# Attention and two mixing blocks in one launch: ScalarE makes both bias tables, TensorE gets idle products, one load goes to ScalarE's queue

## The reference

```python
scores = scale * q @ k.T                       # scale = 1/8
keep   = is_global | is_local                  # key < 8, or 0 <= rel < 96
dist   = where(is_global & ~is_local, n_local, abs(rel))
bias   = -slopes[h] * dist                     # slopes[h] = 2 ** -(h + 1) for 8 heads
a      = softmax(where(keep, scores + bias, -1e9))
x      = a @ v                                 # (2, 768, 512) over all heads
u  = x + (V.T @ (U.T @ x))                     # mixing along the sequence, rank 32
x  = u + relu(u @ w_ch1) @ w_ch2               # 512 -> 2048 -> 512
h  = relu(x @ w_in); gate, vv = halves(h)      # 512 -> 1024
out = (gate * (w_spatial @ norm(vv) + b)) @ w_out
```

## Time and profile before

| | us |
|---|---|
| Median of three runs | 530.94 |
| Lowest and highest | 528.90 and 530.97 |
| The profiled execution | 530.2 |
| Its span | 528.4 |
| PE busy | 515.6 |
| DVE busy | 191.3 |
| ACT busy | 181.7 |
| POOL busy | 125.4 |

### The profile page before, as it was taken

One profiled execution on the slowest core, in us unless ns is written; L12 is line 12 of the kernel. 1 busy time (PEld: TensorE's weight loads), 2 busy tenths in 40 slices (PEclk: granted clock), 3 DMA queues, 4 the chain that ended last, 5 costly groups with the idle time before them and its releaser, 6 DMA issues.

```text
span 528.4 us, 7432 instructions
## 1 busy us (share of the span) xinstructions
PE 515.6 (98%) x2808; PEld 440.7 (83%) x2808; DVE 191.3 (36%) x538; ACT 181.7 (34%) x446; POOL 125.4 (24%) x120
## 2 busy tenths in 40 slices
PE   4999999999999999999999999999999999999997
PEld 4799979888788888888888888888888998888996
DVE  6566667722123423121111312112375355440440
ACT  4677788742323321021101233222443212332121
POOL 6477678334333500000000043323000000000000
PEclk8599999999999999999999999999999999999999
DMA  8540641003223210000000022230000000110002
GB/s 241 179 137 2 198 163 42 2 5 117 81 87 111 81 40 1 0 1 1 1 0 1 0 81 89 60 120 19 1 1 2 0 1 0 61 40 21 1 20 99
DMA packets 12245, 27.85 MB, mean 53 GB/s; under 512 B 2225, under 2 KB 2225, under 8 KB 12209
## 3 DMA queue, kind: packets, MB, share of 16 engines
q1 hardware_dynamic: 10480, 24.22, 14.2%
q10 hardware_dynamic: 1728, 3.15, 1.6%
HBM read 24.22 MB, written 3.15 MB: 52 GB/s over the span
## 4 chain that ended last, share of the span: by engine, by line
PE 94%; POOL 2%; DVE 1%; issue 1%; DMA 1%; ACT 0%; DVEq 0%; POOLq 0%; ACTq 0%
PE bank L988 28%; PE bank L1175 25%; PE bank L1163 25%; PE bank L1038 7%; PE bank L1008 4%; PE bank L1021 3%; PE bank L1045 1%; POOL w_slot L421 1%; DVE bias L495 1%; PE bank L1070 1%; PE bank L1059 1%; DMA cfg_i<-in_cfg 1%; POOL qk_split L382 0%; ACT prob L787 0%; DVE qk_split L492 0%
## 5 line engine op out<-in xcount | busy, mean ns | idle before, releaser
L1175 PE MATMUL bank<-hid,w_slot 128*128 128x512 f32 x576 | 139.2, 390 | 0.0
L1163 PE MATMUL bank<-u_split,w_slot 128*128 128x512 f32 x576 | 138.4, 389 | 0.0
L1175 PEld LDWEIGHTS bank<-hid,w_slot 128*128 128x128 f32 x576 | 107.7, 188 | 23.2 <-issue 0.9
L1163 PEld LDWEIGHTS bank<-u_split,w_slot 128*128 128x128 f32 x576 | 107.7, 188 | 22.4
L659 DVE SCALAR_TENSOR_TENSOR hid<-bank,hid 128x512 fp32r<-128x512 f32 x48 | 33.2, 691 | 192.3 <-ACT hid L885 192.3
L885 ACT ACTIVATE hid<-bank 128x512 fp32r<-128x512 f32 x48 | 28.7, 598 | 203.4 <-PE bank L1163 203.4
L787 ACT ACTIVATE prob<-prob,row_min 128x256 f32<-128x256 f32 (+1 forms) x96 | 45.8, 479 | 18.4 <-DVE row_min L510 18.4
L421 POOL TENSOR_TENSOR w_slot<-stage,w_slot 128x1024 fp32r<-128x1024 f32 x16 | 38.2, 2388 | 52.3 <-ACT w_slot L841 52.3
L988 PE MATMUL bank<-sp_slot,vn 128*128 128x384 f32 x288 | 50.3, 334 | 0.0
L988 PEld LDWEIGHTS bank<-sp_slot,vn 128*128 128x128 f32 x288 | 50.0, 188 | 0.2
L1038 PEld LDWEIGHTS bank<-v_all,probT 128*128 128x128 f32 x352 | 43.2, 198 | 2.6 <-issue 1.8
(11 more groups left out here) (89 smaller groups left out, 455.7 us busy)
## 6 DMA issues: line engine op xcount, KB each, us to landing
stage<-in_w_ch SPq DMA_DIRECT2D x16, 512.0 KB, 3.3
qk_raw<-in_qk SPq DMA_DIRECT2D x24, 256.0 KB, 4.5
v_all<-in_v SPq DMA_DIRECT2D x12, 256.0 KB, 5.1
out_dram<-o_stage ACTq DMA_DIRECT2D x12, 256.0 KB, 2.0
stage<-in_w_spT SPq DMA_DIRECT2D x6, 384.0 KB, 3.0
stage<-in_w_in SPq DMA_DIRECT2D x4, 512.0 KB, 3.3
stage<-in_w_out SPq DMA_DIRECT2D x2, 512.0 KB, 3.5
V_raw<-in_V SPq DMA_DIRECT2D x4, 96.0 KB, 4.1
```

The lines of the kernel that those rows point to most:

```text
L1163: last = mm(h_bank[g % 2][:], w_slot[f][:, a, k * P:(k + 1) * P], u_split[c][:, m, k, :], start=(k == 0 and p == 0), stop=(k == KD - 1 and ...
L1175: last = mm(c_ring[(KD * c + k) % 6][:], w_slot[f][:, a, 512 + k * P:512 + (k + 1) * P], hid[g % 2][:, m, :], start=(f == 0 and a == HI an ...
```

## The change

1. ACT makes `bias0` too (eight activations with `dist0` as input), each with its own signal `bias0_set`. DVE does only the two splits. 2. ACT makes the wide `bias` tables two at a time inside its loop: heads 0 and 1 ahead of `exps(0)`, 2 and 3 behind `exps(1)`, 4 and 5 ahead of `exps(2)`, 6 and 7 ahead of `exps(3)`. `score_bias` waits for the tables that it reads. 3. PE does five idle products ahead of `turn(0)` and two more between its pairs. 4. The first half of q and k of block 0 is loaded from ACT's queue as ACT's first instruction, ahead of the table load, and no longer from SP's.

```diff
@@ sync
-                for hq in range(2):
+                for hq in range(1 if t == 0 else 0, 2):
                     c = slice(2 * hq, 2 * hq + 2)
                     sp.dma_start(qk_raw[r][:, c, :, :], qk[t, :, c, :, :]).then_inc(qk_in[r][hq], 16)
@@ vector
-            vec.tensor_scalar(dist[:, 0:GLOB], far[:, 0:GLOB], n_local, None, ALU.add).then_inc(dist_set, 1)
+            vec.tensor_scalar(dist[:, 0:GLOB], far[:, 0:GLOB], n_local, None, ALU.add)
             dve.drain()
             vec.tensor_copy(dist0[:, GLOB:], dist[:, P + GLOB:])
-            vec.tensor_tensor(dist0[:, 0:GLOB], dist[:, P:P + GLOB], dist[:, 0:GLOB], ALU.min)
-            dve.drain()
+            vec.tensor_tensor(dist0[:, 0:GLOB], dist[:, P:P + GLOB], dist[:, 0:GLOB], ALU.min).then_inc(dist0_set, 1)
             for hq in range(2):
                 c = slice(2 * hq, 2 * hq + 2)
                 dve.wait_ge(qk0_hi, hq + 1)
                 vec.tensor_tensor(qk_split[:, LO, c, :, 0:P], qk_raw[0][:, c, :, :],
                                   qk_split[:, HI, c, :, 0:P].bitcast(F32), ALU.subtract).then_inc(qk0_lo, 1)
-                for h in range(4 * hq, 4 * hq + 4):
-                    vec.tensor_scalar(bias0[:, h, :], dist0[:], -(2.0 ** -(h + 1)) / SCALE, None, ALU.mult)
-            dve.drain()
             def score_bias(g):
-                if g == 2:
-                    dve.wait_ge(bias_set, 1)
                 dve.wait_ge(scored, g + 1)
                 for m in range(2):
+                    if g < 2:
+                        dve.wait_ge(bias0_set, heads(g, m)[1][1] + 1)
+                    elif g < 4:
+                        dve.wait_ge(bias_set, heads(g, m)[1][1] + 1)
@@ scalar
+            act.dma_start(qk_raw[0][:, 0:2, :, :], qk[0, :, 0:2, :, :]).then_inc(qk_in[0][0], 16)
             act.wait_ge(ident_set, 2)
             sc.activation(tiny[:, 0:1], ident[:, 0:1], ACT.Exp)
...
-            act.wait_ge(dist_set, 1)
+            act.wait_ge(dist0_set, 1)
             for h in range(H):
-                last = sc.activation(bias[:, h, :], dist[:], ACT.Copy, scale=-(2.0 ** -(h + 1)) / SCALE)
-            last.then_inc(bias_set, 1)
+                sc.activation(bias0[:, h, :], dist0[:], ACT.Copy, scale=-(2.0 ** -(h + 1)) / SCALE
+                              ).then_inc(bias0_set, 1)
+
+            def set_bias(first):
+                for h in range(first, first + 2):
+                    sc.activation(bias[:, h, :], dist[:], ACT.Copy, scale=-(2.0 ** -(h + 1)) / SCALE
+                                  ).then_inc(bias_set, 1)
...
+                    if s in (-2, 0, 1):
+                        set_bias((0, None, 4, 6)[s + 2])
                     if 0 <= s + 2 < QUADS:
                         exps(s + 2)
+                    if s == -1:
+                        set_bias(2)
@@ tensor
-            for _ in range(WARM):
-                mm(aux[:, 0:P], ident[:], ident[:], start=True, stop=True)
+            def fill(count):
+                for _ in range(count):
+                    mm(aux[:, 0:P], ident[:], ident[:], start=True, stop=True)
+            fill(WARM)
...
             def turn(g):
                 for m in range(2):
+                    if g == 0 and m == 1:
+                        fill(2)
                     pe.wait_ge(expd, 2 * g + m + 1)
...
                 for s in range(-2, QUADS):
+                    if s == 0:
+                        fill(5)
```

More of the change, by code:

```diff
@@ L155, in build @@
         cfg_in, b_in, U_in, V_in = [sem(n) for n in ("cfg_in", "b_in", "U_in", "V_in")]
-        counted, V_round, fold_set, dist_set = sem("counted"), sem("V_round"), sem("fold_set"), sem("dist_set")
+        counted, V_round, fold_set = sem("counted"), sem("V_round"), sem("fold_set")
         z_some, z_copy = sem("z_some"), sem("z_copy")
+        dist0_set, bias0_set = sem("dist0_set"), sem("bias0_set")
         bias_set, iotas, ident_set, V_split = sem("bias_set"), sem("iotas"), sem("ident_set"), sem("V_split")
```

## The result

The changed kernel takes 522.28 us (four runs, 522.26 to 522.32) against 530.96 for the kernel before (528.90 to 530.99): 8.7 us less, a ratio of 0.984 with a 95% interval of 0.982 to 0.986. I had forecast 524.9 and a range of 523.4 to 529.0.

The account below looks back on a forecast made before the run. PE was taken to bound the kernel, leaving its start and clock to gain: 3.5 us from the start plus 3.0 from the clock, less 0.3 for `cfg`, is 6.2; 524.7 on the runs' scale, taken as 524.9, range 523.4 to 529.0.

Parts of the forecast that it names:

- The first exponential: Start of ACT's exponentials: moves from 12.88 to 9.4 us, a gain of 3.5 us (bounds 2.4 to 4.3).
- the branch on ACT is hidden in the trace of before; DVE's 1.59 is the nearest row: Reading two numbers and branching ahead of the wide tables: priced at 1.59 us, bounds 1.0 and 2.0.
- The start of ACT's tables: ACT's narrow tables start at 5.4 us, when `dist0` is ready, and end at 7.1 after 1.7 us.
- The second split behind POOL: In rival "The start gains little" (chance 0.18): DVE's second split waits for POOL's subtraction, first exponential gains 2.3, 529.0 us.
- The first load: Block 0's load on ACT's queue: issues 0.43 us earlier, gains nothing; delays `cfg` by 0.3 us (0 to 0.8).
- The stages 0 to 2: With a high clock ACT bounds them; `turn(3)` starts at 21.8 instead of 28.32 us, a gain of 6.5.
- The 0.45 for the two products at the low clock: Idle products between `turn(0)`'s pairs: at the low clock they take 0.78 us and lose 0.45.
- The clock: PE's clock stays high for most of stages 0 to 2, 3.0 us of the gain; forecast case, chance 0.43.
- short stretch at the low level: A short low-clock stretch is likely somewhere, so 524.9 us was taken instead of 524.7.
- The clock falls again: Rival, chance 0.33: low clock in the first stages as before, gain 3.05 to 5, about 526.8 us.
- the two reasons given for a high clock: Ahead of `turn(0)`: 1.1 to 1.9 us of dense idle products; PE's pause shrinks from 5.14 to under 1.5 us.
- The slower case: Rival, chance 0.06: ACT's added work leaves PE gaps in stages 0 to 3, clock rises late; 533.6 us.

Follow-up runs that it names:

- The two drain experiments: Changed kernel with drains of VectorE and ScalarE ahead of the branch: 523.65 us; kernel before without VectorE's drain, a signal per narrow table instead: 529.11 us.
- the runs of 532.5 and 524.5 us at a high clock: Kernel before plus seven idle products, one run of ten: 532.5 us; changed kernel with all wide tables ahead of the first exponential, one of four: 524.48 us.

## Why the prediction was wrong in size

*The first exponential: mis-sized by the branch.* The step that failed is "the branch on ACT is hidden in the trace of before; DVE's 1.59 is the nearest row". DVE's row was measured behind a drain; both new queues have none, and the sequencer does the reading and branching beside the running instructions, so the term is nothing. Both bounds that I kept, 1.0 and 2.0, left zero out. The two drain experiments show it from both sides: with drains the first exponential comes 1.5 us later and the time grows by 1.4, and in the kernel before it comes 1.2 us earlier without one, with 1.6 us less between the last table and the scored heads.

*The start of ACT's tables: wrong the other way.* The first exponential came at 8.26 us instead of 9.4, 1.15 us and not 1.6 sooner, because a second error hid a part of the first. I let the tables start at 5.4, when `dist0` is ready, and wrote that `dist0` comes behind both casts of ACT. It comes behind their starts only: the second cast began at 5.32 us and the wide tables at 5.85. In the changed kernel the tables go on from the second cast at about 6.0, so this term was 0.6 us too small. The rest of that sum held: a narrow table on ACT takes 1.69 / 8 = 0.21 us, two wide ones 0.61. The gain of 4.6 us lies above my bounds for it, 2.4 to 4.3.

*The second split behind POOL: did not happen, but it can.* In the changed kernel the two splits took 1.36 us side by side, with no table between, and POOL's copy beside the second took 1.08 us instead of 0.6. In the kernel before with seven products the second split began after POOL's subtraction and was held up as that rival said:

```profile
7.00 1.76 DVE L492 TENSOR_TENSOR qk_split<-qk_raw,qk_split 128x512 fp32r<-128x512 f32 x1
```
```profile
6.94 1.27 POOL L382 TENSOR_TENSOR qk_split<-qk_raw,qk_split 128x512 fp32r<-128x512 f32 x1
```

It took 1.76 us with 22 products too, and 1.09 with eleven, against 0.69 alone. So the rival's mechanism exists, and what the change altered is the order: with the two splits side by side, ahead of POOL's first subtraction, the wait appears in none of the eight traces that have them so (1.29 to 1.42 us for both).

*The first load: right in the sum, wrong in the place.* No gain, and `cfg` 0.2 us late. As ACT was busy with its second cast until 6.03, that lateness did not reach the chain. What did is the second half of block 0, which I had taken to land sooner and which landed later, at the head of the chain, by about 0.2 us. It is inside the 8.26, so the 0.3 that I took off for `cfg` was too much.

*The stages 0 to 2: right in kind.* From the first exponential to `turn(3)` I had 12.4 us and 12.05 came, ACT being the bound as worked out; the missing 0.35 are mostly `add_eps` and the two `take_probT`, which take 0.09, 0.27 and 0.28 of the chain where I had 0.25, 0.36 and 0.36. ACT's instructions overlap a little when it never waits (`take_probT` runs from 12.19 to 12.55 us and `add_eps` starts at 12.45), so the step from start to start counts. The 0.45 for the two products at the low clock was not needed; where the clock was low they took 0.85 and cost about 0.8.

*The clock: right, and I took away too much.* PEclk never fell in the first 22 us, so the "short stretch at the low level" (0.2) was not there. And I had added 0.7 us since the profiled run before was that much faster than the median. The gain of 8.0 us was read between two profiles, and the result follows the profiled run before: 530.2 less 7.9 is 522.3. Why that run was 0.7 us faster is not shown; its mean clock, 0.983, is that of the runs at 531. What is seen is that the four runs of the changed kernel lie within 0.06 us and that the kernel before scatters by over 2. At the very start the low level has to be read from durations: PEclk shows 1.00 there too, but until 4.7 us an idle product's record takes 421 ns, the same as at 0.50 in the kernel with 22 products, and 275 after that. So a mean clock of 1.00 leaves this start out.

Together: 524.9 less 1.15, 0.35, 0.3, 0.2 and 0.7 is 522.2.

*The rivals.* "The clock falls again" is what happens without the idle products (525.6), so it was a near thing and not a remote one, and of the two reasons given for a high clock the shorter pause alone did not hold it. The slower case did not arise; in the kernels where the clock was low PE was the bound, as argued.

What stays open: why the products in the kernel before hold the clock in some runs only, why it was high in one run without any, and the runs of 532.5 and 524.5 us at a high clock.

## What to carry to other kernels

Price a wait from a row that stands behind the same kind of instruction: here a read and branch behind a drain cost over a us, the same one in an open queue nothing. When a queue's next term starts, take the last end of what stands ahead of it on that queue, not only the arrival of its input. In a pause of PE that can't be closed, idle products are worth trying, in the number that fills it at the low rate: seven in a long pause paid only now and then, eleven in most runs, 22 held up the work. Before adding a difference between one profile and the median to a forecast, ask what makes it, and whether the change removes that.

## What the runs showed of the hardware

- Reading two numbers from memory and branching, on ACT: 1.26 us from 7.79 to 9.05 behind a drain; without one it leaves no gap between the queued activations (eight tables in 1.69 us, while the second number was read at 6.25).
- An issue on a second queue does not come free for its neighbours: with a 256 KB load issued at 0.75 us on ACT's queue, a 2 KB one issued on SP's at the same time is first used 0.2 to 0.6 us later, and the cast of the next 256 KB one, though that is issued 0.4 us sooner, starts at 5.42 to 5.55 us against 5.01 to 5.32 (seven traces each).
- A VectorE operation of 0.69 us that starts behind GpSimd's subtraction takes 1.76 us; two of them side by side, ahead of the subtraction, take 1.36 together, and GpSimd's copy beside the second 1.08 instead of 0.6.
- One narrow table (128x128, float32) beside a busy POOL takes from 0.21 to 1.30 us on DVE, and 0.21 on ACT, the mean of eight (1.69 us).
- The same binary's time goes with the stretch at the low clock, but not exactly: the kernel with eleven products takes 531.0 us at a mean of 0.987 and 526.3 to 527.4 at 0.993 to 1.000; the one with seven took 532.5 once at 0.999.
- A pause of TensorE of 1.42 us without idle products was followed by the low clock (0.50 from 10 us), one of 1.45 us behind five of them was not (1.00).
